# Three half row buffers and 274-column sum/difference matmuls in the transform stage of an FFT + two-layer MoE kernel

## The chip, the cores and the metric

The kernel runs on one core of one Trainium2 chip. The metric is the device time of one execution in microseconds (us), taken on the core. Lower is better.

## The reference, cut to what matters

```python
X = fft(fft(x, axis=1), axis=2).real          # x: 8 batches of 3072 x 256, f32
x = X.reshape(8 * 3072, 256)
# layer 1: experts chosen by normalised rows against normalised embeddings
logits = (x / (norm(x) + 1e-6)) @ (emb / (norm(emb) + 1e-6)).T / tau      # 8 experts
e = argmax(logits); gate = softmax(logits)[e]
x = gate * (relu(x @ w1[e]) @ w2[e])                                      # 256 -> 1024 -> 256
# layer 2: the same with logits = x @ w_gate
```

The real part of a row and of its mirror row (k and 3072 - k) have the same ingredients: if a row's two partial products are A and B, one row is A + B and the other A - B. Each of them is only computed for 129 of its 256 columns; the norm over the 256 values is the same for both rows of a mirror pair.

## The kernel before, in words

The kernel has two stages. The **transform stage** (the first 500 us) computes the rows of all eight batches, chooses each row's expert and writes every row as a record of 258 floats (256 values, the gate's denominator, the token number) into an HBM table sorted by expert. The **expert stage** (all the rest) runs the two layers over tiles of that table. Only the transform stage is touched by the change.

The transform stage works on one batch at a time, and each engine has its own program, held together by counting semaphores:

- **VectorE (DVE)** computes butterflies of the input for half 0 and half 1 of the columns (`butterflies(h, b)`, L529 to L591: four operations of 1024 columns, two of 1536, then shorter ones), and inside them the low parts of the expert weights (`low_part`, L522). Its `combine` (L593) reads A and B of each of 12 row tiles from the buffer `ab` in SBUF and writes A + B (L603) and A - B (L604) into the row buffer `yrec`, 24 slots of 128 rows. `route` (L613) has three parts: 0 makes logits, maxima and the one-hot choice (L629 to L644); 1 scales by the norms (L647 to L651); 2 takes the exponentials' sums, writes gate and token into `yrec`, and makes from the ranks the row numbers `dest` (L654 to L670). Its order for a batch is: butterflies 0 of the next batch, combine, route part 0, butterflies 1 of the next batch with route parts 1 and 2 slipped in after its 4th and 6th operation.
- **TensorE (PE)** runs, for each batch, `first_transform(0)` (L750; 6 pairs of classes into three banks `vbank`), `turn_weights` (L725, 16 transposes in four groups into three banks `rbank`), `first_transform(1)`, `second_transform` (L782; for each of 12 row tiles A and B as 137-column matmuls, L791: 48 matmuls, which the profile counts as 96 passes), `gate_weights` (L738, L746) and `ranks` (L800, L804 and L807).
- **ScalarE (ACT)** copies results from PSUM: `vt` (L871), `w_turned` (L867), `ab` (L890, one activation of 274 columns for each row tile), the high parts of the weights (`high_part`, L840 and L847, that wait for a load of `raw`), two squares with a sum for each row tile (L884, 24 for a batch), the square root (L902) and the exponential (L858). Each of the last two is preceded by a table load.
- **GpSimd (POOL)** waits for `dest` and then issues 24 indirect DMAs for a batch (L503), one for each slot of `yrec`, which scatter the rows into the record table.
- **SyncE (SP)** issues loads of `xin` (the next batch's input) and `raw` and the stores of the weights' split parts in one fixed order (L347 to L415).

What orders the work around the change is the single row buffer: `combine` of a batch has to wait, quarter by quarter, until the scatter of the batch before has landed (L599):

```python
if 2 * i % QUARTER == 0 and not (isinstance(b, int) and b == 0):
    dve.wait_ge(scattered[2 * i // QUARTER], b * (16 * QUARTER))
```

and PE's `ranks(b)` stands at the end of a batch, ahead of the next `first_transform(0)`, and waits for route part 0 (L803). `turn_weights` waits before its fourth group for ACT to have copied its first (L730, L731), as both use the same bank. PE's `first_transform(h, b)` waits for `butterflies(h, b)` (L755).

Of the kernel before, what the change touches and what calls it, by code (L numbers as in the profile page):

```python
# [5 lines left out]
SEQ, DIM = 3072, 256  # L6
P = 128
J = SEQ // P
HALF = DIM // 2
E = 8  # L10
ROWTILES = 12
SLOTS = 2 * ROWTILES
QUARTER = SLOTS // 4
# [12 lines left out]
SQUARES_LAG = 6  # L26
# [26 lines left out]
def transform_and_experts(nc, x, emb, tau, weights, w_gate, fmat, rowmat, fullmat, tokens, ident_in, tri_in,  # L53
# [136 lines left out]
    with ctx:  # L190
# [38 lines left out]
        with ExitStack() as sa:  # L229
# [28 lines left out]
            sumsq = sb("sumsq", [P, SLOTS], f32, sa)  # L258
# [38 lines left out]
            ab_used = sem("ab_used", sa)  # L297
            combined = sem("combined", sa)
# [4 lines left out]
            scattered = [sem(f"scattered{k}", sa) for k in range(4)]  # L303
# [25 lines left out]
            CB = 2 * ROWTILES + 1  # L329
            RT = 21  # L330
            block = sa.enter_context(nc.Block())

            QP = 8 * PARTS

# [6 lines left out]
            def _(sp):  # L341
# [60 lines left out]
                for c in range(2):  # L402
                    sp.dma_start(rowm[:, c, :, 0:HALF + 1], rowmat[c * P:(c + 1) * P, :, :]).then_inc(rest_in, 16)
# [86 lines left out]
            def _(pool):  # L490
# [7 lines left out]
                with pool.Fori(0, B) as b:  # L498

                    pool.wait_ge(routing, b * RT + RT)  # L500
                    pool.sem_inc(stores_begun, 1)
                    for s in range(SLOTS):
                        pool.indirect_dma_start(records[0], bass.IndirectOffsetOnAxis(dest[:, s:s + 1], 0),  # L503
                                                yrec[:, s, :], None, bounds_check=ROWS - 1,
                                                oob_is_err=False).then_inc(scattered[s // QUARTER], 16)
                for k in range(4):
                    pool.wait_ge(scattered[k], B * (16 * QUARTER))

            @block.vector
            def _(dve):  # L510
# [18 lines left out]
                def butterflies(h, batch, prior, between=None):  # L529
# [28 lines left out]
                    low_part(batch, 4 * h)  # L558

# [13 lines left out]
                    low_part(batch, 4 * h + 1)  # L573
                    dve.wait_ge(butterfly, prior + 10)
# [7 lines left out]
                    low_part(batch, 4 * h + 2)  # L582
                    dve.wait_ge(butterfly, prior + 16)
# [7 lines left out]
                    low_part(batch, 4 * h + 3)  # L591

                def combine(b):  # L593


                    for i in range(ROWTILES):
                        if 2 * i % QUARTER == 0 and not (isinstance(b, int) and b == 0):

                            dve.wait_ge(scattered[2 * i // QUARTER], b * (16 * QUARTER))  # L599
                        dve.wait_ge(rows_evacuated, b * ROWTILES + i + 4)  # L600
                        A, Bm = (view(ab[:, i, s, :], 0, [(1, 2), (1, HALF)]) for s in range(2))
                        y = yrec[:, 2 * i, :]
                        nc.vector.tensor_tensor(view(y, 0, [(REC + HALF, 2), (1, HALF)]), A, Bm, ALU.add).then_inc(combined, 1)  # L603
                        nc.vector.tensor_tensor(view(y, REC, [(HALF - REC, 2), (1, HALF)]), A, Bm, ALU.subtract).then_inc(combined, 1)  # L604

                    dve.wait_ge(mid_row_evacuated, b + 2)
                    dve.wait_ge(combined, b * CB + CB - 1)
                    nc.vector.tensor_copy(view(yrec[0:1, SLOTS - 1, :], 0, [(HALF, 2), (1, HALF)]),
                                          view(ab_mid[0:1, :], 0, [(1, 2), (1, HALF)])).then_inc(combined, 1)
# [3 lines left out]
                def route(b, part):  # L613


                    count = [(0, 8, 11)[part]]
# [7 lines left out]
                    L = HALF + 1  # L624
# [834 lines left out]
```

## Time and profile before

| what | value |
|---|---|
| time, median of 3 runs | 2927.88 us (2925.6 to 2928.78) |
| the profiled execution's own time | 2932.91 us |
| its span | 2930.9 us |
| transform stage: last `dest` made | 500.3 us |
| first matmul of the expert stage | 545.4 us |
| busy share of the span, PE, DVE, ACT, POOL | 92%, 45%, 40%, 21% |
| TensorE's granted clock in six slices of 60 us between 59 and 416 us | 0.85, 0.86, 0.83, 0.83, 0.80, 0.80 |

The profiled execution took 5.0 us more than the median of the runs; 2.0 us of its time lie outside its span. How to read it: the shares over the whole span say little about the transform stage, because 2390 of the 2931 us are the expert stage, where PE is busy all the time at full clock. In the transform stage the granted clock is a mean over stretches at full clock (2.4 GHz) and at half of it (1.2 GHz). A timeline row gives the start, the time from the start of its first to the end of its last instruction, the engine, the line, the operation, its tiles and shapes, a count, and in brackets the idle time before it with what ended it. Instructions overlap in an engine's pipeline, so the distance from one start to the next is often shorter than a duration. Matmuls of 32-bit data appear as two passes each.

### The profile page before, as it was taken

What the parts mean: (1) busy time and instruction counts of PE and PEld (TensorE: products, weight loads), DVE (VectorE), ACT (ScalarE), POOL (GpSimd) and SP (SyncE); (2) the same over time, 40 slices, a digit from 0 to 9 for tenths busy, and PEclk for the clock granted to TensorE, in tenths of its full rate; (3) what the DMA queues carried; (4) which work ended last, traced back from release to release, by engine and by line L of the source; (5) the groups of instructions that cost most, each with busy time, mean ns of one, the idle gap of its engine ahead of it and who ended that gap; (6) DMA issues with size and microseconds to landing.
All of it is one profiled execution on the core that took longest, in us unless ns stands there. A gap on an engine that the chain in (4) does not pass through costs nothing. (4 is left out here: it accounts for less than half of the span.)

```text
span 2930.9 us, 69456 instructions
## 1 busy us (share of the span) xinstructions
PE 2694.9 (92%) x22938; PEld 2439.7 (83%) x22938; DVE 1324.1 (45%) x3980; ACT 1168.4 (40%) x2543; POOL 628.2 (21%) x639
## 2 busy tenths in 40 slices
PE   6777776599999999999999969999999999999998
PEld 5666675499988998989989958999899898998997
DVE  8888875244544544545445433332323232332332
ACT  3554454243443434434444323333333333333332
POOL 2345544211111111111111111111111111111111
PEclk9888787799999999999999989999999999999999
DMA  9567764436354545353635242253341523154230
GB/s 284 159 174 215 195 187 133 130 95 225 111 184 156 182 139 194 102 192 92 216 116 192 64 124 71 79 184 131 126 139 50 193 73 123 54 201 142 76 105 28
DMA packets 250221, 412.78 MB, mean 141 GB/s; under 512 B 41355, under 2 KB 192672, under 8 KB 236705
## 3 DMA queue, kind: packets, MB, share of 16 engines
q1 hardware_dynamic: 221568, 332.60, 36.6%
q0 software_dynamic: 28320, 75.94, 7.5%
q8 instruction: 187, 3.06, 0.4%
q14 instruction: 146, 1.19, 0.1%
HBM read 776.27 MB, written 133.29 MB: 310 GB/s over the span
## 5 line engine op out<-in xcount | busy, mean ns | idle before, releaser
L1141 DVE SCALAR_TENSOR_TENSOR m_hT_low<-m_hbank,m_hT_high 128x512 bf16<-128x512 f32 (+1 forms) x824 | 554.1, 673 | 1401.6 <-ACT m_hT_high L1254 1401.6
L1323 PE MATMUL m_hbank<-m_xT_low,up_high 128*128 128x256 bf16 (+1 forms) x3296 | 761.1, 274 | 0.0
L1325 PE MATMUL m_hbank<-m_xT_top,up_low 128*128 128x256 bf16 (+1 forms) x3296 | 751.2, 271 | 0.0
L1343 PE MATMUL m_ybank<-down_high,m_hT_low 128*128 128x264 bf16 (+1 forms) x3184 | 732.7, 278 | 0.0
L1345 PE MATMUL m_ybank<-down_low,m_hT_high 128*128 128x264 bf16 (+1 forms) x3184 | 728.8, 272 | 0.0
L1254 ACT ACTIVATE m_hT_high<-m_hbank 128x512 fp32r<-128x512 f32 (+1 forms) x824 | 480.2, 583 | 597.6 <-PE m_hbank L1325 597.4
L1320 PE MATMUL m_hbank<-m_xT_high,up_high 128*128 128x256 f32 (+1 forms) x3296 | 592.8, 302 | 22.9 <-issue 17.0
L1286 ACT ACTIVATE m_yr<-m_ybank,m_meta 128x264 f32<-128x264 f32 (+1 forms) x398 | 169.0, 474 | 782.9 <-PE m_ybank L1345 782.8
L1320 PEld LDWEIGHTS m_hbank<-m_xT_high,up_high 128*128 128x128 f32 x3296 | 446.8, 191 | 37.0 <-issue 19.2
L1340 PE MATMUL m_ybank<-down_high,m_hT_high 128*128 128x264 f32 (+1 forms) x3184 | 432.5, 288 | 1.0 <-issue 1.0
L1114 POOL DMA_INDIRECT records<-m_yr,m_idx x199 | 193.5, 972 | 1012.7 <-DVE m_idx L1199 964.4
L1114 POOL DMA_INDIRECT out<-m_yr,m_idx x199 | 193.5, 973 | 990.4 <-ACT m_yr L1286 949.5
L1340 PEld LDWEIGHTS m_ybank<-down_high,m_hT_high 128*128 128x128 f32 x3184 | 394.5, 189 | 1.2 <-issue 1.2
L1323 PEld LDWEIGHTS m_hbank<-m_xT_low,up_high 128*128 128x128 bf16 x3296 | 322.7, 98 | 63.3
L1343 PEld LDWEIGHTS m_ybank<-down_high,m_hT_low 128*128 128x128 bf16 x3184 | 304.6, 96 | 66.9
L1325 PEld LDWEIGHTS m_hbank<-m_xT_top,up_low 128*128 128x128 bf16 x3296 | 326.6, 99 | 27.7
L1345 PEld LDWEIGHTS m_ybank<-down_low,m_hT_high 128*128 128x128 bf16 x3184 | 309.4, 97 | 42.9
L503 POOL DMA_INDIRECT records<-yrec,dest x192 | 224.8, 1171 | 262.7 <-DVE dest L670 157.9
L1302 PE MATMUL m_xbank<-ident,m_xt 128*128 128x128 f32 x796 | 125.2, 279 | 56.6 <-DMA m_xt<-records 56.6
L1129 DVE TENSOR_TENSOR m_xT_low<-m_xbank,m_xT_high 128x512 bf16<-128x512 f32 x206 | 137.0, 665 | 61.8 <-ACT m_xT_high L1244 61.8
L764 PE MATMUL vbank<-fm,arena 128*128 128x256 f32 x352 | 123.4, 436 | 43.9 <-DVE arena L589 43.9
L1244 ACT ACTIVATE m_xT_high<-m_xbank 128x512 fp32r<-128x512 f32 x206 | 119.5, 580 | 72.5 <-PE m_xbank L1302 71.5
(194 smaller groups left out, 2204.0 us busy)
## 6 DMA issues: line engine op xcount, KB each, us to landing
up_high<-w_high SPq DMA_DIRECT2D x210, 1024.0 KB, 6.5
down_high<-w_high SPq DMA_DIRECT2D x103, 1056.0 KB
up_low<-w_low SPq DMA_DIRECT2D x210, 512.0 KB, 7.6
down_high<-w_high SPq DMA_DIRECT2D x104, 1024.0 KB, 5.5
down_low<-w_low SPq DMA_DIRECT2D x103, 528.0 KB
down_low<-w_low SPq DMA_DIRECT2D x104, 512.0 KB, 6.7
m_xt<-records SPq DMA_DIRECT2D x192, 258.0 KB, 3.0
m_raw<-in_weights SPq DMA_DIRECT2D x66, 249.0 KB, 3.0
```

What stands on the lines that cost most here:

```text
L503: pool.indirect_dma_start(records[0], bass.IndirectOffsetOnAxis(dest[:, s:s + 1], 0), yrec[:, s, :], None, bounds_check=ROWS - 1, oob_is_e ...
L1114: pool.indirect_dma_start(target, bass.IndirectOffsetOnAxis(idx[:, j % 4, s:s + 1], 0), yr[:, j % 4, s, lead:lead + width], None, bounds_c ...
L1129: nc.vector.tensor_tensor(xT_low[:, :, 0:w], xbank[:].rearrange("p (c t) -> p c t", c=2)[:, :, 0:w], xT_high[:, :, 0:w].bitcast(f32), ALU. ...
L1141: nc.vector.scalar_tensor_tensor(hT_low[:, j % 2, 2 * i:2 * i + 2, 0:w], hbank[i][:].rearrange("p (c t) -> p c t", c=2)[:, :, 0:w], 0.0, h ...
L1254: nc.scalar.activation(hT_high[:, j % 2, 2 * i:2 * i + 2, 0:w], hbank[i][:].rearrange("p (c t) -> p c t", c=2)[:, :, 0:w], ACT.Relu).then_ ...
L1286: y = nc.scalar.activation(yr[:, j % 4, s, 0:step_w], ybank[s][:, 0:step_w], ACT.Copy, scale=meta[:, j % 4, s, 0:1])
L1320: nc.tensor.matmul(h, up_high[:, j % 2, at:at + P], xT_high[:, c, 0:w], start=(f == 2 * i and c == 0), stop=False, skip_group_check=True)
L1323: nc.tensor.matmul(h, top_half(up_high[:, j % 2, at:at + P]), xT_low[:, c, 0:w], start=False, stop=False, skip_group_check=True)
L1325: done = nc.tensor.matmul(h, up_low[:, j % 2, at:at + P], xT_top[:, c, 0:w], start=False, stop=(c == 1), skip_group_check=True)
L1340: nc.tensor.matmul(y, hT_high[:, j % 2, c, rows], down_high[:, j % 2, cols], start=(c == 0), stop=False, skip_group_check=True)
L1343: nc.tensor.matmul(y, hT_low[:, j % 2, c, rows], top_half(down_high[:, j % 2, cols]), start=False, stop=False, skip_group_check=True)
L1345: done = nc.tensor.matmul(y, top_half(hT_high[:, j % 2, c, rows]), down_low[:, j % 2, cols], start=False, stop=(c == FC - 1), skip_group_c ...
```

## The change

- **Row matmuls.** For each row tile the moving operand is now `[row matrix, row matrix]` or `[row matrix, -row matrix]`, 274 columns wide. All four matmuls of a tile add up in one region of a bank, which then holds A + B and A - B. GpSimd builds the copy and the negated copy once, after `build_slots`; the first `second_transform` waits for it (`rowm_ready`).
- **ScalarE writes the rows.** `ab` and `combine` are gone. For each tile ACT copies A + B, A - B and the logits from PSUM in three activations. ACT squares one row of each mirror pair, 13 squares instead of 24, all after the copy of the gate weights; two square roots spread them over 24 slots.
- **Three half row buffers.** `yrec` has 36 slots, three halves of 12. Half n of the sequence (batch b has halves 2b and 2b + 1) uses buffer n mod 3. ACT waits before a batch's row tiles 0 and 6 until the half that used the buffer before is scattered (halves 2b - 3 and 2b - 2).
- **Later routing.** Route part 0 of batch b stands in butterflies 1 of batch b + 1, after its 16th operation; part 1 behind those butterflies; part 2 in butterflies 0 of batch b + 2, after its 10th operation, where DVE also waits for the whole scatter of batch b - 1 before it overwrites `dest`. PE's `ranks(b)` stands ahead of the 4th pair of `first_transform(0, b + 1)`, and ACT's exponentials of b behind its copy of that transform's 5th pair.
- **Weights.** For b > 0 PE runs `turn_weights(b)` ahead of `first_transform(0, b)`, and ACT copies the result first in a batch. ACT makes high parts 0 to 3 of the next batch during `first_transform(0)` and high parts 4 to 7 during the last four row tiles; for batch 0 all eight stand ahead of the transform.
- **Unrolled.** The batch loops of DVE, PE, ACT and POOL are written out; SP's loop is as it was.

The diff, cut:

```diff
-            rowm = sb("rowm", [P, 2, 2, NCOL], f32, sa)
-            ab = sb("ab", [P, ROWTILES, 2, NCOL], f32, sa)
-            ab_mid = sb("ab_mid", [1, NCOL], f32, sa)
-            yrec = sb("yrec", [P, SLOTS, REC], f32, sa)
+            rowm = sb("rowm", [P, 2, 2, 2, NCOL], f32, sa)
+            yrec = sb("yrec", [P, 3 * HALFSLOTS, REC], f32, sa)
...
+            ROUTE2_AT, ROUTE0_AT, RANKS_AT, EXPS_AT = 4, 5, 3, 4
+            def slot(b, s):
+                return (2 * b + s // HALFSLOTS) % 3 * HALFSLOTS + s % HALFSLOTS
+            def wait_half(eng, n):
+                if n >= 0:
+                    eng.wait_ge(scattered[n % 3], HALF_STORED * (n // 3 + 1))
...
 # GpSimd, behind build_slots
+                nc.gpsimd.tensor_copy(rowm[:, :, 0, 1, :], rowm[:, :, 0, 0, :]).then_inc(rowm_ready, 1)
+                nc.gpsimd.tensor_scalar(rowm[:, :, 1, 1, :], rowm[:, :, 1, 0, :], -1.0, None, ALU.mult).then_inc(rowm_ready, 1)
...
 # VectorE
-                def finish(b):
-                    butterflies(0, b + 1, b * (2 * BF) + 2 * BF)
-                    combine(b)
-                    route(b, 0)
-                    butterflies(1, b + 1, b * (2 * BF) + 3 * BF, lambda n: route(b, n))
+                for b in range(B - 1):
+                    butterflies(0, b + 1, b * (2 * BF) + 2 * BF, lambda n: gates(b - 1, n))
+                    butterflies(1, b + 1, b * (2 * BF) + 3 * BF, lambda n: rows(b, n))
+                    route(b, 1)
+                route(B - 2, 2)
+                gate_low(B - 1)
                 for part in range(3):
                     route(B - 1, part)
...
 # VectorE, route part 2
+                        wait_half(dve, 2 * b - 2)
+                        wait_half(dve, 2 * b - 1)
                         step(nc.vector.tensor_copy(dest[:], first[:]))
...
 # TensorE, first_transform
                     for pair in range(6):
+                        if h == 0 and pair == RANKS_AT and b > 0:
+                            ranks(b - 1)
 # TensorE, second_transform
-                                last = nc.tensor.matmul(bank[:, s * NCOL:(s + 1) * NCOL], vt[h][:, at:at + P], rowm[:, h, s, :],
-                                                        start=(h == 0), stop=(h == 1))
+                                last = nc.tensor.matmul(bank[:, 0:2 * NCOL], vt[h][:, at:at + P],
+                                                        rowm[:, h, s, :, :].rearrange("p a n -> p (a n)"),
+                                                        start=(s == 0 and h == 0), stop=(s == 1 and h == 1))
...
-                def transform(b):
+                for b in range(B):
+                    if b > 0:
+                        turn_weights(b)
                     first_transform(0, b)
-                    turn_weights(b)
+                    if b == 0:
+                        turn_weights(b)
                     first_transform(1, b)
                     second_transform(b)
                     gate_weights(b)
-                    ranks(b)
+                ranks(B - 1)
...
 # ScalarE, the row tiles (transform(b) stands ahead of rows(b))
+                        if i == 0:
+                            wait_half(act, 2 * b - 3)
+                            if b > 0:
+                                act.wait_ge(routing, (b - 1) * RT + 6)
+                        if i == ROWTILES // 2:
+                            wait_half(act, 2 * b - 2)
+                        bank, y = rbank[i % 3][:, :], yrec[:, slot(b, 2 * i), :]
+                        nc.scalar.activation(view(y, 0, [(REC + HALF, 2), (1, HALF)]), view(bank, 0, [(1, 2), (1, HALF)]), ACT.Copy)
+                        nc.scalar.activation(view(y, REC, [(HALF - REC, 2), (1, HALF)]), view(bank, NCOL, [(1, 2), (1, HALF)]), ACT.Copy)
+                        nc.scalar.activation(logits[:, 2 * i:2 * i + 2, :], view(bank, L, [(NCOL, 2), (1, E)]),
                                              ACT.Copy).then_inc(rows_evacuated, 1)
+                        if i >= ROWTILES - 4 and b + 1 < B:
+                            high_part(b + 1, i - ROWTILES + 8)
...
+                    for n in range(SQ):
+                        square(b, n)
+                    nc.scalar.activation(norm[:, SLOTS - 2:SLOTS], sumsq[:, ROWTILES - 1:SQ], ACT.Sqrt).then_inc(norms_ready, 1)
+                    nc.scalar.activation(norm[:, 0:SLOTS - 2].rearrange("p (i s) -> p i s", s=2),
+                                         sumsq[:, 0:ROWTILES - 1, None].to_broadcast([P, ROWTILES - 1, 2]), ACT.Sqrt).then_inc(norms_ready, 1)
-                for q in range(4):
+                for q in range(8):
                     high_part(0, q)
```

## Rows read from the trace of the kernel before

**Rows 1.** Timeline of PE: the gate weights of batch 0 and of batch 7.
```profile
71.39 4.46 PE L746 MATMUL mbank<-wg,w_turned 128*128 128x8 f32 x32
...
488.15 4.77 PE L746 MATMUL mbank<-wg,w_turned 128*128 128x8 f32 x32
```

**Rows 2.** Waits between 100 and 480 us: us in total, times, longest us.
```profile
DVE yrec L603 <- DMA records<-yrec,dest: 36.9, 9, 6.2
```

**Rows 3.** Timeline of PE, 204 to 262 us: batch 3, last line ranks(3).
```profile
204.69 0.59 PE L764 MATMUL vbank<-fm,arena 128*128 128x256 f32 x2
205.12 0.59 PE L765 MATMUL vbank<-fm,arena 128*128 128x256 f32 x2
...
213.47 2.00 PE L734 MATMUL rbank<-ident,raw 128*128 128x128 f32 x16 [0.28 <-PE midbank L777]
221.28 1.22 PE L764 MATMUL vbank<-fm,arena 128*128 128x256 f32 x2 [5.81 <-DVE arena L589]
...
232.84 0.28 PE L777 MATMUL midbank<-fm,arena 128*128 128x1 f32 x2
235.64 11.45 PE L791 MATMUL rbank<-rowm,vt 128*128 128x137 f32 x96 [2.52 <-ACT vt L871]
...
247.57 3.74 PE L746 MATMUL mbank<-wg,w_turned 128*128 128x8 f32 x32
...
259.41 2.23 PE L807 MATMUL mbank<-onehot,ones_bf 128*128 128x192 bf16 x24
```

**Rows 4.** Timeline of DVE over the same time: route of batch 2, combine of batch 3.
```profile
204.19 0.17 DVE L647 TENSOR_SCALAR rnorm<-norm 128x24 f32<-128x24 f32 x1
...
209.44 0.35 DVE L654 TENSOR_REDUCE gsum<-expd 128x24 f32<-128x192 f32 x1 [1.01 <-ACT expd L858]
...
211.59 0.18 DVE L670 CAST dest<-first 128x24 int32<-128x24 f32 x1
...
221.67 1.22 DVE L541 TENSOR_TENSOR tsum<-xin 128x1024 f32<-128x1024 f32 x1
...
234.00 0.55 DVE L577 TENSOR_TENSOR arena<-tsum 128x384 f32<-128x384 f32 x1
...
254.06 0.43 DVE L603 TENSOR_TENSOR yrec<-ab 128x256 f32<-128x256 f32 x1 [5.46 <-DMA records<-yrec,dest]
```

**Rows 5.** Timeline of ACT: 209 to 214 us, then the end of batch 4.
```profile
209.04 0.36 ACT L858 ACTIVATE expd<-shifted 128x192 f32<-128x192 f32 x1
...
213.10 0.60 ACT L871 ACTIVATE vt<-vbank 128x512 f32<-128x512 f32 x1 [0.71 <-PE vbank L770]
...
315.53 0.22 ACT L898 ACTIVATE wg_high<-mbank 128x64 fp32r<-128x64 f32 x1 [2.17 <-PE mbank L746]
...
320.61 1.28 ACT L902 ACT_TABLE_LOAD   x1
321.90 0.22 ACT L902 ACTIVATE norm<-sumsq 128x24 f32<-128x24 f32 x1
```

**Rows 6.** Timeline of POOL (batches 2 and 7) and the landing of its DMAs.
```profile
212.66 1.63 POOL L503 DMA_INDIRECT records<-yrec,dest  x1 [24.58 <-DVE dest L670]
...
221.83 1.90 POOL L503 DMA_INDIRECT records<-yrec,dest  x1 [0.30 <-issue]
...
231.04 1.48 POOL L503 DMA_INDIRECT records<-yrec,dest  x1 [0.30 <-issue]
...
501.22 0.97 POOL L503 DMA_INDIRECT records<-yrec,dest  x1 [14.09 <-DVE dest L670]
...
DMA to landing us min/median/max: 4.6/4.9/5.3
```

**Rows 7.** Timelines of ACT in batch 0 and of DVE in batch 7.
```profile
38.59 0.63 ACT L847 ACTIVATE high<-raw 128x512 fp32r<-128x512 f32 x1 [0.29 <-DMA raw<-in_weights]
...
54.55 0.63 ACT L847 ACTIVATE high<-raw 128x512 fp32r<-128x512 f32 x1 [2.01 <-DMA raw<-in_weights]
...
500.16 0.18 DVE L670 CAST dest<-first 128x24 int32<-128x24 f32 x1
```

More of the change, by code:

```diff
@@ L25 @@
 DEPTH = 4
[L26 removed]
+HALFSLOTS = SLOTS // 2
 NCOL = HALF + 1 + E
@@ L302, in transform_and_experts @@
             routing = sem("routing", sa)
-            scattered = [sem(f"scattered{k}", sa) for k in range(4)]
+            scattered = [sem(f"scattered{k}", sa) for k in range(3)]
             stores_begun = sem("stores_begun", sa)
@@ L558, in butterflies @@
                     low_part(batch, 4 * h)
+                    between(3)
                     dve.wait_ge(planes_used[h], batch + 1)
@@ L591, in butterflies, with gate_low @@
                     low_part(batch, 4 * h + 3)
[L593 to L609, printed above, removed]
+                    between(6)
+                def gate_low(b):
                     dve.wait_ge(wg_high_done, b + 1)
@@ L657, in route @@
                         settle()
-                        step(nc.vector.reciprocal(yrec[:, :, GATE], rnorm[:]))
-                        step(nc.vector.tensor_copy(yrec[:, :, TOKEN], token_ids[:]))
-                        step(nc.vector.tensor_scalar_add(token_ids[:], token_ids[:], float(SEQ)))
+                        for a in range(2):
+                            at, rows = slot(b, a * HALFSLOTS), slice(a * HALFSLOTS, (a + 1) * HALFSLOTS)
+                            step(nc.vector.reciprocal(yrec[:, at:at + HALFSLOTS, GATE], rnorm[:, rows]))
+                            step(nc.vector.tensor_copy(yrec[:, at:at + HALFSLOTS, TOKEN], token_ids[:, rows]))
                         dve.wait_ge(ranks_ready, b + 1)
@@ L683, in _, with gates, rows @@
                 dve.wait_ge(prep_v, 8)
-                dve.sem_inc(ab_used, 1)
                 butterflies(1, 0, BF)
-                def finish(b):
-                    butterflies(0, b + 1, b * (2 * BF) + 2 * BF)
-                    combine(b)
-                    route(b, 0)
-                    butterflies(1, b + 1, b * (2 * BF) + 3 * BF, lambda n: route(b, n))
-                finish(0)
-                with dve.Fori(1, B - 1) as b:
-                    finish(b)
-                combine(B - 1)
+                def gates(b, n):
+                    if b >= 0 and n == ROUTE2_AT:
+                        route(b, 2)
+                def rows(b, n):
+                    if n == ROUTE0_AT:
+                        gate_low(b)
+                        route(b, 0)
+                for b in range(B - 1):
[4 more added lines that the diff above has]
+                gate_low(B - 1)
                 for part in range(3):
@@ L816, in transform @@
                     gate_weights(b)
-                    ranks(b)
-                transform(0)
-                with pe.Fori(1, B) as b:
-                    transform(b)
+                ranks(B - 1)
                 sum_steps(pe, tab, tab_summed, table_sums)
@@ L871, in body @@
                             nc.scalar.activation(vt[h][:, pair * 512:(pair + 1) * 512], vbank[pair % 3][:], ACT.Copy).then_inc(v_evacuated, 1)
-                            if pair < 4:
-                                high_ahead(b, h, pair, last)
-                            if h == 0 and pair == 1 and not first:
+                            if h == (b == 0) and pair < 4 and b + 1 < B:
+                                high_part(b + 1, pair)
+                            if h == 0 and pair == EXPS_AT and b > 0:
                                 gate_exps(b - 1)
@@ L896, in body @@
+                    nc.scalar.activation(view(yrec[0:1, slot(b, SLOTS - 1), :], 0, [(HALF, 2), (1, HALF)]),
+                                         view(midbank[0:1, :], 0, [(1, 2), (1, HALF)]), ACT.Copy)
+                    nc.scalar.activation(logits[0:1, SLOTS - 1, :], midbank[0:1, L:NCOL], ACT.Copy).then_inc(mid_row_evacuated, 1)
                     act.wait_ge(wg_ready, b + 1)
```

107 lines of the change are left out of this document (49 added, 58 removed).

## The prediction

> **What bounds the kernel now.** I read the page's busy shares by slice first: the expert stage is PE at full clock and not touched, so only the transform stage up to about 545 us counts. There no engine is full, so the next view is the list of waits. The reader should see that DVE's sum rows waited 36.9 us for scatters to land, in 9 waits between 100 and 480 us [rows 2], and that PE's waits in the timeline end on DVE's butterflies (5.81 us) or ACT's copies (2.52 us) [rows 3]. Followed in time, it is a ring. `dest` is made at 211.77, POOL starts 0.9 us later and needs 36.5 us for 24 issues, the last quarter lands and frees `combine` at 254.06 [rows 4, 6], then come route part 0, the next butterflies, exponentials and `dest` again. From the end of the gate weights of batch 0 (75.85) to that of batch 7 (492.92) there are 417.1 us [rows 1], **59.6 us for a batch**. Below, T is the moment when PE ends a batch's gate weights.
>
> **The new second transform.** A 256-column f32 matmul (two passes) takes 0.43 us from start to start (204.69 to 205.12) and 96 passes of 137 columns 11.45 us [rows 3]. For 274 columns a matmul is 0.4325 x 274/256 = 0.463 us, and 48 of them 22.2 us: **+10.75 us for a batch** on PE, and nothing hides it once PE is the last.
>
> **What goes.** `combine` costs DVE 24 operations of 0.43 us a batch (254.06 [rows 4]), some 9 us as they overlap a little, and its 36.9 us of waits go. I price this at nothing: DVE has slack in the new order (below). Eleven squares and the 274-column copy go from ACT, three copies a tile come. ACT takes 0.36 us for 192 columns [rows 5], so two copies of 256 and one of 16 cost a tile under 1.2 us, against 1.85 us that PE needs for a tile: hidden as long as PE's tile is the longer. GpSimd's two copies of the row matrices (once) and the unrolled loops: nothing (POOL has no other work until the first `dest`; batch 0 was unrolled before too). If POOL were late with them, the first rows would wait once.
>
> **The ring of PE and ACT.** From T, ACT makes the gate copy, 13 squares, the roots, and only then the copy of turned weights that PE's fourth group of transposes needs. In batch 4, gate copy to table load was 5.08 us with 12 squares [rows 5]; one more at 0.4 makes 5.5. Table load 1.3, two roots 0.4, first copy 0.6 [rows 5]: T + 7.8. PE did three of the four groups (2.00 us for all [rows 3]) by T + 1.5 and stands still for **6.3 us**, a stall that was not there before, as `turn_weights` used to follow the first transform. Fourth group: T + 8.3. First transform 0 after a standstill runs partly at 1.2 GHz: after 5.81 us of idleness the first two passes took 1.22 us instead of 0.59, and the whole 221.28 to 233.12 = 11.85 us [rows 3]: T + 20.15. Ranks 2.3 (row of 2.23): T + 22.4. First transform 1 now follows without a gap, at full clock: 22 x 0.43 + 0.7 = 10.2: T + 32.6. Copy of the last pair 0.6 [rows 5]: T + 33.2. Rows 22.2, middle row 0.5, gate weights 3.75 [rows 3]: **T + 59.7**.
>
> **The ring of the scatter.** Roots at T + 7.2, route part 1 0.85: T + 8.05. Butterflies 0 up to the 10th operation take 12.3 us (221.67 to 234.00) [rows 4]: DVE is there at T + 20.4, but the exponentials are not. They stand behind the fifth pair: 8.3 + 1.6 (low clock) + 5 x 1.73 + 2.3 (ranks) = 20.85, copy 0.5, table load 1.3, exponential 0.36 [rows 5]: T + 23.0. Route part 2 took 209.44 to 211.77 = 2.35 us [rows 4], with two more small operations 2.6: `dest` at T + 25.6, POOL at T + 26.5. The first half of 12 issues took 212.66 to 232.52 = 19.9 us [rows 6]. Lower bound: 12 x (0.97 + 0.30) = 15.2, the rate in batch 7 [rows 6]. An issue takes 1.90 us when DVE starts its 1024-column operations (POOL 221.83, DVE 221.67) and 0.97 when DVE is idle [rows 4, 6]. In the new order DVE works for only 14 us after `dest` (rest of butterflies 0, six operations of butterflies 1) and then waits for ACT's high parts at row tile 8. So 8 issues at the old mean of 1.66 and 4 at 1.27: 18.0. The Trainium skill, SBUF — State Buffer, section Who interferes with whom, says that a DVE instruction with two SBUF inputs contends with a GpSimd instruction that reads SBUF. By that rule the half speeds up when DVE idles and the ring is the 60.2 below; were the issue times set by their place in the series, as one could also read them, it would be 62.1. Landing 4.9 (4.6 to 5.3) [rows 6], so tile 6 can be written at T + 49.5; with 0.75 for its copies PE's tile 9 starts at T + 50.2 (PE holds three tiles in its banks). Three tiles 5.55, then 0.5 + 3.75: **T + 60.1**. The two rings are equal within their error. I take 60.2 for the six periods that have both, and 59.7 for the last, where DVE is idle behind the butterflies and POOL runs at 1.27. DVE's own ring (T + 23.0, 2.6 of route part 2, about 6 of the rest, then 12.3 [rows 4] and 3 more up to route part 0: some 47) stays below.
>
> **The ends.** Batch 0: the rows add 10.75. All eight high parts stand ahead of ACT's first copy of a pair; the last is bound by its load and starts at 38.59 [rows 7], so PE, with three banks full, waits, and three pairs, a waking and four groups of transposes come after 39.8: done at 48.5, where the second first transform could start at 46.4. SP stores the fifth weight piece only after a transpose, and the loads behind it already made ACT wait (2.01 us at 54.55 [rows 7]). All told +4.6 us (0 if the loads catch up, 6 if all is passed on). T of batch 0: 75.85 + 10.75 + 4.6 = 91.2. T of batch 7: 91.2 + 6 x 60.2 + 59.7 = 512.1. Then roots 7.2, exponentials 1.7, route part 2 2.6: `dest` at T + 11.5 = 523.6, against 500.34 before [rows 7]. Behind it 24 issues at 1.27 and the expert stage are as they were.
>
> **Sum:** +23.3 us. Against the profiled execution's 2932.9 this is 2956; it stood 5.0 above the median of 2927.9, so the median becomes **2951 us**. A measurement can tell about 0.2% (5.9 us) from no change.
>
> **The rivals.**
> - **The scatter is late.** If the first half keeps its 19.9 us, or loads make ACT's exponentials late by 2 us, the ring is 62.1 and six periods cost 11 more: 2963. For it: the two rings are equal already, and DMA waits of ACT (2.01) exist. Against it: loads and scatter overlap less in the new order, and batch 7's rate.
> - **The clock falls in the rows.** PE's wait for tile 9 or before the rows brings 1.2 GHz for a part of 22.2 us, up to 2.5 a batch: 2969. For it: the stage's granted clock was 0.80 to 0.86. Against it: PE now works from T + 8 to T + 59.7 almost without a gap, so it has fewer wakings than before.
> - **ACT's tail does not stop PE (faster).** Place: the fourth group of `turn_weights`. If the squares were done in time, the standstill of 6.3 us would go; exponentials, `dest` and the scatter then move up with it and both rings are near 53.8: 2951 - 7 x 6.3 = 2907. It decides from a standstill below 3.0 us (23.3 / 7 = 3.3 a batch less); at about 3.0 the result is no change. For it: the removed waits are real, and PE's clock gains. Against it: ACT's order is written out, and 13 x 0.4 + 1.3 are from rows.
> - **The change breaks even.** Half of ACT's tail is hidden, a standstill of 2.2 to 3.8 us, by the same working: 2922 to 2934.
>
> **How the numbers follow.** Forecast 0.60, late scatter 0.22, clock 0.09, tail hidden 0.05, even 0.04. The time is the forecast's. Its own range: both rings at 59.2 and nothing at the start gives -6 - 4.6 - 1 = 2939 or so; all the upper bounds of the late scatter plus some of the clock give 2968. Range 2939 to 2968, which leaves out the last two cases and the clock at its worst. Faster by over 0.2%: 0.05. Within: 0.04. Slower: 0.91.
>
> **What would show it.** The 96 passes at 22.2 us a batch. PE idle some 6 us ahead of the fourth group of transposes, released by ACT's w_turned. DVE's wait for ACT's exponentials about 3 us, no wait of DVE on a scatter. ACT's row copy of tile 6 with a wait on the scatter of 0 to 3 us. T of batch 0 near 91, of batch 7 near 512, `dest` near 524. Wrong would be: passes shorter than 0.23 us, no idleness of PE at the weights, or a wait of ACT on the scatter above 4 us.

## The result and the profile after

The changed kernel takes **2951.36 us** (median of four, 2948.99 to 2953.23) against 2928.13 for the kernel before: ratio 1.0081, 95% interval 1.0063 to 1.0098. That is 23 us slower; the forecast was 2951. Its profiled execution took 2952.9 us (span 2950.9), 20.0 more than that of before.

The first two parts of the page: busy time by engine, and the busy tenths of 40 slices of 74 us, of which the first seven are the transform stage.

```profile
PE 2762.4 (94%) x22938; PEld 2476.7 (84%) x22938; DVE 1250.9 (42%) x3772; ACT 1173.8 (40%) x2575; POOL 619.5 (21%) x641
...
PE   5988998299999999999999988999999999999998
...
PEclk9998999599999999999999998999999999999999
```

PE's slices in the transform stage, behind the first, are now 8 and 9, nearly without a hole, and this doesn't help: the work in them grew. The mean granted clock rose from 0.955 to 0.966. The timeline of PE over one period, from the gate weights of batch 3 to those of batch 4 (start, us, engine, line, operation, count, idle time before and what ended it):

```profile
270.98 3.74 PE L747 MATMUL mbank<-wg,w_turned 128*128 128x8 f32 x32
274.57 1.90 PE L735 MATMUL rbank<-ident,raw 128*128 128x128 f32 x12
282.40 1.08 PE L735 MATMUL rbank<-ident,raw 128*128 128x128 f32 x4 [5.94 <-ACT w_turned L876]
283.29 1.06 PE L767 MATMUL vbank<-fm,arena 128*128 128x256 f32 x2
...
289.79 1.27 PE L813 MATMUL mbank<-onehot,ones_bf 128*128 128x192 bf16 x24
...
295.76 0.28 PE L780 MATMUL midbank<-fm,arena 128*128 128x1 f32 x2
...
307.21 22.43 PE L795 MATMUL rbank<-rowm,vt 128*128 128x274 f32 x96 [0.57 <-ACT vt L885]
329.57 0.63 PE L801 MATMUL midbank<-rowm,vt 128*1 128x137 f32 x4
330.13 3.90 PE L747 MATMUL mbank<-wg,w_turned 128*128 128x8 f32 x32
```

Two things to see beside [rows 3]: the 96 row passes take 22.43 us where they took 11.45, and PE stands still for 5.94 us ahead of the fourth group of transposes, where a first transform of before had its wait of 5.81 for DVE. The period is 334.03 - 274.72 = 59.31 us; the seven are 59.14, 59.32, 60.32, 59.31, 60.20, 59.31 and 60.19, mean 59.68 against 59.58. What ends the standstill is in ACT's timeline, the tail of batch 3, with 13 squares between the first line and the second:

```profile
274.75 0.22 ACT L917 ACTIVATE wg_high<-mbank 128x64 fp32r<-128x64 f32 x1 [2.69 <-PE mbank L747]
...
280.17 1.28 ACT L921 ACT_TABLE_LOAD   x1
281.46 0.20 ACT L921 ACTIVATE norm<-sumsq 128x2 f32<-128x2 f32 x1
...
281.68 1.55 ACT L876 ACTIVATE w_turned<-rbank 128x512 f32<-128x512 f32 x3
```

The list of waits between 100 and 490 us (us in total, times, longest) has lost the line of [rows 2], DVE's 36.9 us on the scatters, and has these instead:

```profile
DVE low L538 <- ACT high L853: 56.5, 6, 9.4
...
PE rbank L735 <- ACT w_turned L876: 36.8, 7, 6.1
DVE tsum L575 <- PEq L783: 30.4, 6, 5.8
...
ACT yrec L904 <- DMA records<-yrec,dest: 12.6, 4, 3.2
```

That 36.8 us of PE came where 36.9 us of DVE went is a coincidence: the two engines' waits are not terms of one sum. The sum is PE's own. Between the gate weights of batch 0 and those of batch 7 PE's busy time and its waits fill the whole stretch, before and after. Its waits before in that stretch:

```profile
PE vbank L764 <- DVE arena L589: 40.6, 7, 5.8
PE mbank L804 <- DVE onehot L644: 37.9, 7, 8.0
PE rbank L791 <- ACT vt L871: 18.6, 7, 3.7
```

With 2.0 us of small ones they were 99.1 us. After the change they are 43.0: 36.8 for the turned weights, 4.0 for the copy of the last pair and 2.2 small ones. The whole stretch, first before, then after (length; busy us of PE, PEld, DVE, ACT, POOL; granted clock; DMA share; GB/s):

```profile
75.85:492.92 417.07, 318.00 (x1911) 288.55 (x1911) 332.53 (x641) 213.39 (x655) 201.49 (x168) 0.83 0.63 175
95.94:513.73 417.79, 374.82 (x1911) 318.73 (x1911) 253.17 (x440) 212.86 (x663) 190.97 (x168) 0.91 0.59 175
```

So 56.1 us of PE's waits went and 56.8 us of busy time came. The row matmuls account for 67.2 of these (157.0 us in seven batches, before 89.8), and the rest of PE's work took 10.4 us less, at a granted clock of 0.91 instead of 0.83. What paid for the wide rows is the 78.5 us that PE had waited for DVE, and the new standstill of 36.8 us took about half of that back. DVE's slack now lies in its waits: it waits for ACT's high parts and for PE to give back the planes, the inputs of the first transform that DVE overwrites. ACT's wait for the scatter at row tile 6 is 12.6 us in 4 waits and did not reach PE, which has three banks. Windows over two periods (columns as above):

```profile
214.40:274.72 60.32, 54.37 (x275) 46.18 (x276) 40.94 (x69) 31.11 (x96) 28.00 (x24) 0.92 0.67 194
274.72:334.03 59.31, 52.50 (x274) 44.68 (x274) 40.94 (x69) 31.12 (x96) 27.98 (x25) 0.91 0.66 196
```

PE is at work for some 90% of the period, DVE for 69%, ACT for half. The ends: the gate weights of batch 0 end at 91.64 + 4.30 = 95.94 (before 75.85 [rows 1]), `dest` of batch 7 at 524.90 (before 500.34), so 24.6 us of loss stand ahead of the expert stage; the expert stage, untouched, was 4.4 us shorter in this execution (2381.1 against 2385.5, from its first matmul to the end of the span).

### The profile page after: what moved, and what is told of

The parts are those of the page before. It is cut to its first block and busy times, and to the rows that moved or that the text cites. A ratio compares the mean times of both kernels' runs of the same rounds, so it can differ in the third digit from the quotient of the medians.

```text
span 2950.9 us, 68548 instructions
## 1 busy us (share of the span) xinstructions
PE 2762.4 (94%) x22938; PEld 2476.7 (84%) x22938; DVE 1250.9 (42%) x3772; ACT 1173.8 (40%) x2575; POOL 619.5 (21%) x641
## 5 line engine op out<-in xcount | busy, mean ns | idle before, releaser
L1340 PEld LDWEIGHTS m_hbank<-m_xT_high,up_high 128*128 128x128 f32 x3296 | 446.3, 191 | 36.8 <-issue 19.2
L1345 PEld LDWEIGHTS m_hbank<-m_xT_top,up_low 128*128 128x128 bf16 x3296 | 325.8, 99 | 27.1
L514 POOL DMA_INDIRECT records<-yrec,dest x192 | 214.3, 1116 | 295.8 <-DVE dest L666 239.7
L795 PE MATMUL rbank<-rowm,vt 128*128 128x274 f32 x768 | 181.3, 397 | 5.2 <-ACT vt L885 5.2
L795 PEld LDWEIGHTS rbank<-rowm,vt 128*128 128x128 f32 x768 | 146.1, 191 | 37.7 <-ACT vt L885 5.9
```

The source lines that it names most:

```text
L795: last = nc.tensor.matmul(bank[:, 0:2 * NCOL], vt[h][:, at:at + P], rowm[:, h, s, :, :].rearrange("p a n -> p (a n)"), start=(s == 0 and h ...
L1340: nc.tensor.matmul(h, up_high[:, j % 2, at:at + P], xT_high[:, c, 0:w], start=(f == 2 * i and c == 0), stop=False, skip_group_check=True)
L1345: done = nc.tensor.matmul(h, up_low[:, j % 2, at:at + P], xT_top[:, c, 0:w], start=False, stop=(c == 1), skip_group_check=True)
```

## The experiments

The theory: one ring of PE and ACT sets the period, its row passes (22.4 us) wholly on the path, its standstill of 5 to 6 us a second term that ACT's order makes, and batch 0 pays once for the high parts. The rivals: the scatter sets the period (so that repairs of ACT's order bring nothing), or the unrolled loops or the wider passes cost otherwise than thought. The experiments ran on three chips, four kernels on each; the kernel before took 2967.08 us on the first, 2965.83 on the second and 2918.49 on the third. A kernel's time is a median of several executions, narrow's and before_same's that of a single one.

**inline** (first chip): ACT squares a tile right behind its copies.

```diff
+                        if i >= 1:
+                            square(b, i - 1)
...
-                    for n in range(SQ):
-                        square(b, n)
```

> Changed kernel, but each square follows the next row tile's copies on ScalarE (squares 0 to 10 behind tiles 1 to 11, the last two behind the middle row) instead of all 13 behind the gate copy. Theory (PE and ACT ring, broken by ACT's tail): PE's standstill ahead of the fourth group of transposes shrinks from 5.0 to 6.1 us to about 1 us, dest and scatter move up with it, the distance between gate weights falls from 59.7 to about 53.2 us; dest of batch 7 comes 6 us rather than 11 us after its gate weights; median near 2901 us. Rival (the scatter ring binds): the period stays at 59 to 60 us and ScalarE waits for the scatter at row tile 6 by 6 us more; median 2945 to 2951.

Measured: 2979.36 us, 1.0039 of before (1.0025 to 1.0053). The standstill shrank to 1.4 us or less and `dest` of batch 7 came 6.4 us behind the gate weights instead of 11.2, but the periods were 61 to 65 us, the last 77.4, longer than the changed kernel's on the chip of the result, and the time missed the 2901 expected. On this chip the kernel before is 39 us slower, so that without the changed kernel beside it the run doesn't decide; the third chip does.

**turn_first** (first chip): the copies of the turned weights stand ahead of the squares.

```diff
                     nc.scalar.activation(wg_high[:], wg_bank, ACT.Copy).then_inc(wg_high_done, 1)
+                    if b + 1 < B:
+                        weights_turned(b + 1)
                     for n in range(SQ):
```

> Changed kernel, but ScalarE copies the next batch's turned weights ahead of the 13 squares and the roots. Theory: PE gets past the transposes at once but runs into its three full banks, as ScalarE's squares and roots then delay the first pair copies to 10.4 us after the gate weights; PE's ring would be 54.6 us, but the roots, butterflies and dest do not move up, so the scatter ring of about 57.8 us takes over in six periods: median near 2935 us. Rival (only PE's standstill counts): 54.6 us a period, 2916 us. Rival (nothing gained, the wait only moves to the pair copies): 2948 to 2951 us.

Measured: 2983.19 us, 1.0056 (1.0039 to 1.0073), periods 61.0 to 62.4, the last 73.5. PE's wait for the turned weights is gone. The wait moved: DVE waited 35.5 us for ACT's roots (14.7 in after_same), which now stand behind the copies of the turned weights as well as behind the squares.

**narrow** (first chip): the row matmuls at 137 columns, as before the change; A and B themselves are written in place of sum and difference.

```diff
-                                last = nc.tensor.matmul(bank[:, 0:2 * NCOL], vt[h][:, at:at + P],
-                                                        rowm[:, h, s, :, :].rearrange("p a n -> p (a n)"),
-                                                        start=(s == 0 and h == 0), stop=(s == 1 and h == 1))
+                                last = nc.tensor.matmul(bank[:, s * NCOL:(s + 1) * NCOL], vt[h][:, at:at + P],
+                                                        rowm[:, h, s, 0, :], start=(h == 0), stop=(h == 1))
```

> Changed kernel with the old 137-column row matmuls: the rows written are A and B instead of sum and difference, so that routing differs and only the transform stage is to be read. Theory (PE ring first, scatter ring close behind): row matmuls fall from 22.4 to 11.5 us a batch, but the period falls only from 59.7 to about 55.5 us, where the scatter binds (ScalarE waits at row tile 6 for the scatter by some 6 us and PE waits with it). If the scatter had slack, the period would be 48.8 us. If the columns were hidden, it would stay at 59.7.

Measured: 2982.67 us, a single execution. Half of the row work went, and the mean period is 65.6 us, against 55.5 expected and 66.5 in after_same below (another chip, with the same time before); most of what the short rows bring is the earlier start (gate weights of batch 0 at 81.9 instead of 95.6). Its list of waits says why:

```profile
ACT yrec L903 <- DMA records<-yrec,dest: 47.3, 6, 8.8
...
PE rbank L735 <- ACT w_turned L875: 36.3, 6, 6.5
...
PE rbank L795 <- ACT logits L905: 34.4, 12, 6.9
```

With short rows the scatter ring binds: ACT waits 7.9 us a batch for it and PE waits behind ACT. The second ring of the prediction is real. How close it lies under the first this run doesn't show, since its period also holds the waits without a name that are described under before_same.

**late_high** (first chip): the second four high parts of batch 0 go back between the copies of the first transform.

```diff
+                            if b == 0 and h == 0 and pair < 4:
+                                high_part(0, 4 + pair)
...
-                for q in range(8):
+                for q in range(4):
```

> Changed kernel, but the high parts 4 to 7 of batch 0 stand behind the first four pair copies of batch 0 again, as before the change. Theory: the start's shift beyond the 10.75 us of columns was these copies; the gate weights of batch 0 end at 87 to 90 us instead of 95.9 and everything behind moves with them: median near 2944 us. Rival (other starts, such as GpSimd's row matrices or the loads, set it): 95 to 96 us and 2951.

Measured: 2995.2 us, 1.0094 (1.0069 to 1.012). The gate weights of batch 0 end at 86.83 (83.09 + 3.74 in PE's timeline), against 95.57 in the control below: the start costs 8.7 us in this order of ACT, of which 6.3 are left at the end (3001.52 - 2995.2, on two chips on which the kernel before takes the same).

**after_same** (second chip): the changed kernel as it is.

> The changed kernel itself, again, as the control for the chip of these runs. The first experiments ran on a chip on which the kernel before took 2967 us instead of 2928, and had no control. If the surplus lies in what both kernels share, the ratio to the kernel before is 1.008 again (1.006 to 1.010). If the changed kernel is more sensitive to such a chip (its code is written out, its scatter ring is as long as its PE ring), the ratio is above 1.010 there and 1.008 only on a chip at 2928.

**before_same** (second chip): the kernel before as it is, for its trace.

> The kernel before itself, one look, to have its trace from the same chip: distance between gate weights 59.6 us and 545 us to the first expert matmul on a chip at 2928 us. On a chip at 2967 us the surplus of 39 us should lie ahead of the first expert matmul (584 us), as the changed variants' expert stages took 2379 to 2383 us there as well.

Measured: 3001.52 us, 1.0122 (1.0105 to 1.0139), and 2965.82 us. The first matmul of the expert stage comes at 584.8 us in before_same, as expected. The changed kernel's ratio is above 1.010, but it was 1.011 on the third chip too, so that the changed kernel suffers more from such a chip isn't shown. Against this control (another chip than the first, but with the same time before) inline is 22 us less, turn_first 18, narrow 19, late_high 6. Both kernels lose in the transform stage: the mean period of before is 65.2 us here and was 59.6, that of the changed kernel 66.5 and was 59.7, while the expert stage takes the same (2379 to 2383 us). Lines of PE and ACT near 510 us in before_same, with POOL's last issue of the batch, and one of ACT in after_same:

```profile
514.05 2.17 PE L791 MATMUL rbank<-rowm,vt 128*128 128x137 f32 x8 [13.37 <-issue]
```
```profile
504.39 0.60 ACT L871 ACTIVATE vt<-vbank 128x512 f32<-128x512 f32 x1 [4.35 <-remote]
511.48 0.60 ACT L871 ACTIVATE vt<-vbank 128x512 f32<-128x512 f32 x1 [6.49 <-remote]
```
```profile
511.02 0.97 POOL L503 DMA_INDIRECT records<-yrec,dest  x1 [0.31 <-issue]
```
```profile
539.21 0.39 ACT L904 ACTIVATE yrec<-rbank 128x256 f32<-128x256 f32 x1 [11.89 <-remote]
```

Such waits, for which the profile names no instruction, are over 1 us in 37 places in before_same (PE 32.8 us in all, ACT 76.2, DVE 18.2) and in 40 in after_same (PE 16.2, ACT 84.1, DVE 10.6); every one of them lies between the first issue of a batch's scatters and the landing of its last. In the traces of both kernels on the chip of the result there is none, nor on the third chip. What stops the engines was not found; POOL's own issues take the same time on these chips (0.97 us with DVE idle). The stops also change what binds: between 100 and 480 us before_same has no wait of DVE on a scatter, where the same kernel had the 36.9 us of [rows 2] on the chip of the result.

**before_wide** (second chip): in the kernel before, every row matmul is issued twice, 192 passes a batch.

```diff
-                            for h in range(2):
+                            for h in (0, 1, 0, 1):
```

> Kernel before with only the doubling of the row matmuls' time: each of the 48 matmuls of a batch is issued twice (192 passes of 137 columns, 22.9 us for 11.45). Theory (columns are hidden only as far as the old scatter wait reaches): gate weights come 11.4 us later, VectorE, which was ready 4.8 us after them, now waits for them, so that a batch gets 6.5 us longer and the ends 11.4 each: about +62 us, ratio 1.021. The change would then owe 39 us of gain to its new order. Rival (PE had idle time enough): +11 us, ratio 1.004. Rival (fully on the path): 8 x 11.4 = 91 us, ratio 1.031.

Measured: 3062.91 us, 1.0328 (1.0311 to 1.0345). That is 97 us more, beside 8 x 11.45 = 91.6 of added passes, but the passes didn't cost 97. The first matmul of the expert stage in before_same and here:

```profile
584.79 1.12 PE L1302 MATMUL m_xbank<-ident,m_xt 128*128 128x128 f32 x4 [40.81 <-DMA m_xt<-records]
```
```profile
663.85 1.12 PE L1302 MATMUL m_xbank<-ident,m_xt 128*128 128x128 f32 x4 [40.68 <-DMA m_xt<-records]
```

The transform stage is 79.1 us longer; the other 17.8 us lie in the expert stage (2397.0 us against 2379.2), which the edit doesn't touch, and nothing here explains them. In the seven periods the row matmuls took 74.5 us more and the periods 69.0 more. So most of the added passes are on the path of the old order, and the result lies between the +62 and the +91 expected. Whether they would hide under the scatter wait this run can't tell: on this chip the kernel before has no such wait (before_same). The size of the sum's largest term rests on the trace of the result, not on this run.

**before_unrolled** (second chip): the loops of PE, ACT, DVE and POOL in the kernel before are written out, as the change does.

```diff
-                with pe.Fori(1, B) as b:
+                for b in range(1, B):
```

> Kernel before with the batch loops of VectorE, TensorE, ScalarE and GpSimd written out and nothing else changed. Theory (unrolled code costs nothing): ratio 1.000, within 0.2%. Rival (each engine's code now comes from memory once for each batch and stalls while the queues are busy): waits of the kind 'issue' or 'remote' of 1 us and more in ScalarE and TensorE, 10 to 40 us in all, ratio up to 1.014.

Measured: 2958.82 us, 0.9977 (0.9968 to 0.9987). Unrolling costs nothing here. That it gains the 7 us, which the prediction had at zero, isn't shown: of the 11.0 us between the profiled spans 5.2 lie in the expert stage, whose loops are the same (2374.0 us against 2379.2).

The last four ran together on the third chip, where the stalls without a name are absent.

**after_again**: the changed kernel.

> Control: the changed kernel once more, beside the next three. On a chip where the kernel before takes 2928 us: 1.008 of it (2951). On one where it takes 2966: 1.012 (3001).

Measured: 2950.06 us, 1.0109 (1.0092 to 1.0126). Its mean period is 59.58 us, PE waits 36.1 us for the turned weights, T of batch 0 is 96.25: the picture of the result.

**inline_again**:

> ACT squares each row tile right behind its copies, so that the roots and the turned weights come early. On a chip at 2928 the ring of PE and ACT binds alone, and by that theory the standstill ahead of the fourth transposes (5 to 6 us, seven times) goes and nothing takes its place: 2951 less 7 x 6 plus what the wait of ACT on the scatter takes back (DVE's dest comes earlier too), 2905 to 2915, ratio 0.992 to 0.996. The rival, that the scatter ring is as long as that of PE and ACT on any chip, gives a wait of ACT on the scatter of 5 us in place of the standstill and 2940 to 2951. On a chip at 2966: 1.004 again.

Measured: 2916.33 us, 0.9994 (0.9985 to 1.0004): **33.7 us less than its control**, and level with the kernel before. The list of waits between 100 and 490 us:

```profile
ACT high L853 <- DMA raw<-in_weights: 47.3, 21, 6.5
...
DVE tsum L575 <- PEq L783: 14.3, 6, 2.9
...
ACT yrec L904 <- DMA records<-yrec,dest: 11.7, 5, 2.9
...
PE vbank L767 <- ACT vt L885: 10.9, 11, 2.1
...
PE rbank L735 <- ACT w_turned L876: 4.0, 4, 1.2
```

The standstill went from 36.1 us to 4.0, the mean period from 59.58 to 55.46. Seven periods bring 28.9 us, the earlier first T 2.4, the earlier `dest` of batch 7 4.8 (6.38 behind T in place of 11.17); that is 36.1 by the two profiled executions, whose spans differ by 36.9. So the scatter did not hold the period near 60 on this chip; the rival (2940 to 2951) is out. In the seven periods PE's waits fell by 22.2 us (42.3 to 20.1) and its busy time by 6.7 (374.8 to 368.1, granted clock 0.91 to 0.96): a standstill also makes the work behind it run partly at the low clock. It fell short of the 42 us expected since the weight loads are late next: ACT waits 47.3 us for them ahead of its high parts (1.5 in the control), and PE waits 10.9 us for the pair copies behind them, a wait that the control doesn't have. ACT's timeline of batch 5 shows it, with the exponentials and a copy queued behind the load:

```profile
331.01 0.63 ACT L853 ACTIVATE high<-raw 128x512 fp32r<-128x512 f32 x1 [6.22 <-DMA raw<-in_weights]
331.55 0.58 ACT L885 ACTIVATE vt<-vbank 128x512 f32<-128x512 f32 x1
...
337.29 0.36 ACT L857 ACTIVATE expd<-shifted 128x192 f32<-128x192 f32 x1
```

**best1**: inline, turn_first and late_high together.

> Squares inline, ACT's copies of the turned weights ahead of the first transform, and at the start the high parts shared between the halves as before. By the theory the three repairs add: on a chip at 2928 7 us less than inline_again for the start (T of batch 0 at 87) and about 1 us a batch for the order of the weights, 2890 to 2903. On a chip at 2966 the scatter ring binds: only the start counts, 2970 (ratio 1.001). The rival (the scatter ring binds everywhere) gives 2933 to 2944 on the first.

Measured: **2910.8 us, 0.9976 (0.9967 to 0.9986)**: faster than both kernels, 7.7 us less than before and 39.3 less than the change. It missed the 2890 to 2903 expected. T of batch 0 is 87.85 (6.0 earlier than in inline_again, 7 expected) and the mean period 55.17. The order of the weights brought 0.3 us a batch, not 1.

**best2**: best1 with route part 2 a step earlier, ranks and exponentials one and two pairs earlier.

```diff
-            ROUTE2_AT, ROUTE0_AT, RANKS_AT, EXPS_AT = 4, 5, 3, 4
+            ROUTE2_AT, ROUTE0_AT, RANKS_AT, EXPS_AT = 3, 5, 2, 2
```

> best1 with route part 2 one step earlier, ahead of DVE's wait for PE's first transform, and the exponentials and ranks two pairs earlier: dest some 4 to 6 us earlier after T. If the scatter ring binds in best1, each batch gets up to 5 us shorter: 25 to 35 us less than best1. If the ring of PE and ACT binds, the same time as best1 within 5 us.

Measured: 2920.32 us, 1.0008 (0.9998 to 1.0017), 9.5 us slower than best1; both expectations missed it (no gain, and more than 5 us away). `dest` came only 2 to 4 us earlier behind T, since the exponentials stand behind a high part whose load is late; DVE, now earlier, waits for them, and PE waits for ACT's copy of the fourth pair, which the table load and the exponential have pushed back:

```profile
DVE gsum L646 <- ACT expd L857: 22.5, 7, 6.1
PE vbank L767 <- ACT vt L885: 18.9, 12, 3.1
```

In best1 these are 10.8 and 12.2 us. Of the 14.5 us that the seven periods grew, 6.1 are PE's waits and 8.4 its busy time, at a granted clock of 0.93 instead of 0.96. A standing place that is early on paper is worth nothing behind a load.

## Why the prediction was right, point by point

- **The row passes**, forecast 22.2 us a batch: 22.43, the mean of seven, and no wait of PE stands behind their start, so they are on the path whole. In the kernel before they took 12.8 us on the mean of the seven and not the 11.45 of the one batch that the prediction read (14.38 in batch 4, part of them at the low clock). The periods were worked out from T, so that this enters only the comparison.
- **The standstill**, forecast 6.3 us before the fourth transposes, from 13 squares, a table load and two roots: 5.04 to 6.10, and 3.76 once, 36.8 in 7. PE went on at T + 7.68 (282.40 - 274.72) where the sum has 7.8. inline_again took 32 of the control's 36 us away.
- **The ring of PE and ACT**, forecast 59.7: rows begin at T + 32.49 (forecast 33.2), T + 59.31 at the end. The first transform 0 with the ranks took 12.75 us instead of 14.15, as the ranks ran at full clock in 1.27 where the row of before had 2.23.
- **The ring of the scatter**, forecast 60.1 to 60.2, didn't bind, and that it came near at all is two errors against each other. The step "`dest` at T + 25.6" failed: the last release is not the exponentials' but PE's, DVE waits up to 5.8 us until the first transform has given back the planes (the line `tsum` <- PEq), a wait that the prediction left out, and `dest` came at T + 27.1 to 28.3 in the six batches of the ring. The sign "DVE's wait for ACT's exponentials about 3 us" was missed with it. And the landing of 4.9 us is no landing of a scatter: the line in [rows 6] comes from the view of the tile `yrec` and counts loads into that buffer at the kernel's start, and the trace of the kernel before has no landing of its scatters. In the changed kernel the scatters took (min, median, max):

```profile
DMA to landing us min/median/max: 2.5/3.3/8.1
```

  These are counted from the start of an issue; the prediction added its 4.9 to the end of one. Tile 6 was written at T + 47.8 (forecast 49.5), 2.8 us behind the start of the half's last issue, and ACT waited for it 3.2 us at most, as said. By the prediction's own sum this makes a scatter ring of 58.4 us, below the 59.3 of PE and ACT.
- **The issue times**: 12 issues took 17.91 to 18.03 us in six batches, forecast 18.0 (its terms, 8 x 1.66 + 4 x 1.27, make 18.4). Two of POOL's issues of batch 2, and what DVE did beside the first:

```profile
252.25 1.96 POOL L514 DMA_INDIRECT records<-yrec,dest  x1 [0.30 <-issue]
...
259.25 0.97 POOL L514 DMA_INDIRECT records<-yrec,dest  x1 [0.30 <-issue]
```
```profile
252.15 1.21 DVE L556 TENSOR_TENSOR xin<-xin,tsum 128x1024 f32<-128x1024 f32 x1
```

  While DVE works an issue takes 0.97 to 1.96 us, with DVE idle 0.97, and in batches 6 and 7, when DVE has no more butterflies, all 24 take 0.97. So the place in the series doesn't set the time. The rule of the Trainium skill (SBUF — State Buffer, section Who interferes with whom), that a DVE instruction with two SBUF inputs contends with a GpSimd instruction that reads SBUF, agrees with this trace: the 1.96 us stand beside such a `TENSOR_TENSOR`. That the issue of an indirect DMA counts as such a GpSimd instruction is shown by these durations alone.
- **The start** is the term that was mis-sized: forecast 4.6 us beside the wider rows, measured 20.1 - 10.75 = 9.3. The step "done at 48.5" nearly held (the transposes begin at 47.32 and the second first transform follows at 49.20), but the loads cost more: in the second half ACT waited 6.78 us for the load of a high part and PE 4.41 us behind it, so that the rows of batch 0 began 7.4 us later than before (66.79 against 59.42). And they took 24.4 us with part of them at the low clock, 12.9 more than the 11.5 of before, where the sum has 10.75. late_high and best1, which share the high parts between the halves again, have T of batch 0 8.7 us earlier than after_same and 6.0 us earlier than inline_again.

```profile
61.24 0.63 ACT L853 ACTIVATE high<-raw 128x512 fp32r<-128x512 f32 x1 [6.78 <-DMA raw<-in_weights]
```

- **The sum**, +23.3: first T +20.1 instead of +15.4, seven periods +0.7 instead of +3.8 (417.8 against 417.1 and 420.9), the tail from T to `dest` +3.7 instead of +4.1; +24.6 in all, and the medians differ by 23.2. The start's 4.7 us too few were made good by the periods' 3.1 too many and by 0.3 in the tail, and the expert stage, 4.4 us shorter in the profiled execution, does the rest. The mechanism is right; that the total agrees within 1 us is luck.
- **The rivals**: a late scatter did not come on the chip of the result; "the tail does not stop PE" is what inline_again made true, and its price there was 33.7 us, where the text had 44; part of the rest went to waits behind the weight loads. The clock did not fall in the rows: they took 22.43 us on the mean. Nor did the change break even, since the standstill was 5.0 to 6.1 us in six of seven. Both halves of the balance can be seen: double the row passes and the kernel before loses 79 us in its transform stage (before_wide, on the chip with the stops), take the new standstill out and the changed kernel is level with the kernel before. That the wide rows cost their full length on an undisturbed chip is read from PE's sum of busy time and waits; no run there tests it alone.

## What to carry to other kernels

When a wait is removed from one ring, work out the next ring in full before counting the gain: here PE's 78.5 us of waits for DVE went, and 67.2 us of wider rows and 36.8 us of waits for ACT's tail came. Count the waits of the engine that the path runs through, and not those of another whose total happens to be near. Moving a combine into matmul columns freed DVE, which was busy for 80% of the seven periods (332.5 of 417.1 us) and now for 61%, and cost PE the columns' full length; what hides that must be named. And the order on the evacuating engine is worth as much as the change: putting each square behind its tile's copy gave back 34 us.

## What the runs showed of the hardware that was not expected

- The transform stage depends on the chip: the same kernel before took 2918.5, 2928.1, 2965.8 and 2967.1 us on four chips, and between the two traced ones (the chip of the result and before_same) all of the difference lies ahead of the expert stage. On the two slower ones PE, ACT and DVE stop for 1 to 13 us without a named releaser, only while indirect scatters are under way. Ratios are steadier than times, but they move too: the change was 1.008, 1.011 and 1.012.
- The kernel with written-out loops was 0.23% faster (before_unrolled), on the second chip alone, and about half of that lies in a stage whose loops are the same.
- The expert stage is the same code for all of these kernels, and its length in the profiled executions is not: 2374.0 us in before_unrolled, 2377 to 2386 in most, 2397.0 in before_wide. A difference of a few microseconds between two such kernels needs its place in the trace before it is given to the edit.
